# A spectral mixer's opening: near rows of the last DFT group summed and mirrored by DVE, the preceding tokens scaled by ACT

## The chip, the cores and the metric

The kernel runs on one core of one Trainium2 chip. The metric is the device time of one execution in microseconds (us); lower is better. The core's engines run side by side and are ordered by semaphores: TensorE (PE, with PEld for its weight loads), VectorE (DVE), ScalarE (ACT), GpSimd (POOL) and SyncE (SP), which issues the transfers here.

## What is computed

An input of 4 sequences of 3072 tokens with 256 channels goes through three stages: the real part of a DFT over tokens and channels, a channel mixing layer in which each token is blended with the one before it, and a routed layer of 8 experts.

```python
X = np.fft.fft(np.fft.fft(x, axis=1), axis=2).real              # 4 x 3072 x 256
x_prev = np.concatenate([zeros(B, 1, D), X[:, :-1, :]], axis=1)
xk = mu_k * X + (1.0 - mu_k) * x_prev
xr = mu_r * X + (1.0 - mu_r) * x_prev
v = np.maximum(xk @ w_k, 0.0) ** 2 @ w_v                         # 256 -> 1024 -> 256
x = sigmoid(xr @ w_r) * v
# then: per token the expert with the largest x @ w_gate, up to 384 tokens
# for each expert in order, out = prob * (relu(x @ w1[e]) @ w2[e])
```

## The kernel before

**Tiles and stages.** The 256 channels lie on 128 partitions in two halves, h = 0 and 1; tokens lie along the free dimension, in the tile `xt`. A sequence is 24 rows (`N2`) of 128 tokens, and a mixing tile is 512 tokens, so 4 rows (`NEAR`) of the sequence, 24 tiles in all. For the first sequence the whole DFT runs ahead of the first tile (`first_dft` of each engine); the DFTs of the other three are cut into pieces that run between the products of the tiles before them.

**Precision.** Matmul operands are float32 values split into a high part (rounded to the format of the fast matmul) and a low part (the rest). A product is three matmuls: high x high, weights' low x high, high x low. ACT makes the high part by copying `raw` to the narrower type (`high_part`, L745), DVE the low part by subtracting (`low_part`, L966).

**The last step of the DFT.** PE multiplies 13 blocks in four groups (`GROUPS3`, `step3`), each into an odd and an even bank. A block gives 5 (`JS`) token positions in each of the 24 rows. ACT copies the odd bank to `odd_copy`; DVE's `sums` (L946) adds it to the even bank for channel half 0 and subtracts for half 1. That gives positions 0 to 64 of each row. The other 63 are mirror images: `mirrors` (L699) on ACT copies half 1's positions in reverse to half 0 of the row at the other end and the reverse. `outer` picks the rows 0 to 3 and 20 to 23 (the near rows: rows 0 to 3 are the first tile, and rows 20 to 23 are their mirror images' sources), `inner` the 16 between. The channel that sits alone at the fold, partition 0 of half 1, comes from a separate small product, and SP writes it into `xt` by DMA (`place_edge`, L489): first its near rows once all near mirrors are done, later the others.

**The first tile.** With the near rows in place, DVE takes the difference between each token and its predecessor (L994, L956), multiplies it by mu and adds the predecessor (L1001, L963); ACT makes the high parts (L735, L737, L748), DVE the low ones (L969). Channel half 0 of xk is done in two halves of 256 tokens so that PE can start early. PE's `opening_ups` (L1404) computes the first four 128-wide blocks of the hidden layer in four banks, block by operand: high parts of xk half 0 (L1411), its low part (L1414), then the gate's products of xr half 0 (L1437), xk half 1 (L1422), and so on to L1430. Before the opening PE fills its wait with products of zeros (L385). After it come `up(4)` and `up(5)`, `down(0)`, `up(6)` and so on: each up writes a block of the hidden layer to a bank that its relu must have left (`hb_drained`), each down adds a block's contribution to the output. ACT's relu of the first block (L773) stands in its queue behind all mirrors of the first sequence. DVE squares what relu leaves (L1086) and makes its low part (L1081), ACT its high part (L768).

**What sets the order.** Each engine's program is written out by hand, and each engine runs it strictly in order; a wait holds everything behind it. Counting semaphores tie them together: `s3_summed` counts sums, `near_mirrored[h]` near mirrors of a half, `x_high` high parts, `mixed` low parts (one ahead), `hb_drained` relus (two ahead).

Of the kernel before, what the change touches and what calls it, by code (L numbers as in the profile page):

```python
# [18 lines left out]
P = 128  # L19
BATCH, SEQ, DIM, FF = 4, 3072, 256, 1024  # L20
EXPERTS, EFF = 8, 1024
N1, N2 = 128, 24
# [4 lines left out]
JS = 5  # L27
# [68 lines left out]
def build(nc, ins, out, cap):  # L96
# [55 lines left out]
    mu_r = ph("mu_r", [P, DH])  # L152
    earlier = ph("earlier", [P, P], bf16)
# [97 lines left out]
    half_dx, half_raw, half_high = sem("half_dx"), sem("half_raw"), sem("half_high")  # L251
# [38 lines left out]
    OPENING = [0, 2, 1, 3]  # L290
# [17 lines left out]
    first_quads, later_quads = [v_pair, h_pair, r_pair, v_pair], [r_pair, v_pair, r_pair, r_pair]  # L308
# [57 lines left out]
    def outer(rows):  # L366

        return rows.rearrange("p (b s) j -> p b s j", s=NEAR)[:, ::N2 // NEAR - 1]

# [107 lines left out]
    with ctx:  # L477
        with nc.Block("main") as block:
# [189 lines left out]
            def _(act):  # L668
# [42 lines left out]
                def first_dft():  # L711
# [191 lines left out]
            def _(dve):  # L903
# [67 lines left out]
                def first_dft():  # L971
# [14 lines left out]
                    for g in range(QUADS - 1):  # L986
                        sums(0, first_quads, g)
                    sums(0, first_quads, QUADS - 1, (1, 0))
                    dve.wait_ge(consts_in, 16 * CONSTS)
                    dve.wait_ge(s3_summed, DH * QUADS)  # L990
                    dve.wait_ge(near_mirrored[0], QUADS)
                    dve.wait_ge(mixed, 1)
                    for k, half in enumerate(HALVES):
                        dx = nc.vector.tensor_tensor(xr_raw[:, 0, half], xt[:, 0, half.start + 1:half.stop + 1], xt[:, 0, half], ALU.subtract)  # L994
                        if k == 0:
                            dx.then_inc(half_dx, 1)
                            dve.wait_ge(half_dx, 1)
                        else:
                            dx.then_inc(dx_ready, 1)
                            dve.wait_ge(dx_ready, 1)  # L1000
                        raw = nc.vector.scalar_tensor_tensor(xk_raw[:, 0, half], xr_raw[:, 0, half], mu_k[:, 0:1], xt[:, 0, half], ALU.mult, ALU.add)  # L1001
                        if k == 0:
                            raw.then_inc(half_raw, 1)
                        else:
                            raw.then_inc(raw_ready, 1)
                    dve.wait_ge(raw_ready, 1)
                    mix(0, OPENING[1], 0)
                    low_part(OPENING[0], 0, 0)
                    dve.wait_ge(near_mirrored[1], QUADS)
                    dve.wait_ge(near_edge_in, 32)  # L1010
                    difference(0, 1, 0)
                    mix(0, OPENING[2], 0)
                    low_part(OPENING[1], 0, 1)
                    low_part(OPENING[2], 0, 2)
                    mix(0, OPENING[3], 0)
                    low_part(OPENING[3], 0, 3)
# [244 lines left out]
            def _(pe):  # L1261
# [34 lines left out]
                def step3(seq, quads, g):  # L1296
# [5 lines left out]
                    for bank, lo, m, full3 in ((odd, 0, m_odd, s3_odd_full), (even, ZO, m_even, s3_even_full)):  # L1302
                        for q in range(*GROUPS3[g]):
                            at = (q - GROUPS3[g][0]) * SCOLS
                            done = mm(bank[:, at:at + SCOLS], z[:, q, lo:lo + P], m, start=True, stop=True)  # L1305
# [11 lines left out]
                def first_dft():  # L1317
# [9 lines left out]
                    for g in range(QUADS):  # L1327
# [6 lines left out]
                        step3(0, first_quads, g)  # L1334
# [6 lines left out]
                def route_rows(m):  # L1341
                    for h in range(DH):
# [313 lines left out]
```

## Time and profile before

| | |
|---|---|
| Median of 3 timed runs | 606.71 us (606.59 to 606.94) |
| The profiled execution | 607.38 us |
| Its span, first to last instruction | 605.5 us |
| PE busy | 595.1 us, 98% |
| DVE busy | 446.8 us, 74% |
| ACT busy | 319.2 us, 53% |
| POOL busy | 102.5 us, 17% |
| Chain that ended last | PE 91%, DMA 3%, DVE 2%, ACT 1% |

Times in rows are microseconds from the span's first instruction. A row of the timeline gives the start, the duration, the engine, the line, the operation, its output and inputs, the shapes, how many instructions are merged in it, and in brackets the engine's idle time before it with what ended it. SPq is a transfer being issued by SyncE. Instructions of one engine overlap a little: the next starts before the last one's end. A float32 product of the DFT is two PE records, as is a product of zeros. A mean over the whole span says little here, since the change touches 15 us of it.

### The profile page before, as it was taken

The numbers are of one execution on the slowest core, as the hardware profiler recorded it, in microseconds if no ns is written. First come the engines' busy times: TensorE is split into PE (matmuls) and PEld (weight loads), VectorE is DVE, ScalarE is ACT, GpSimd is POOL, SyncE is SP. The second block draws the span as 40 slices with busy tenths as digits, with TensorE's granted clock in tenths as the row PEclk, the third lists the DMA queues.
The fourth block names the chain that finished last, engine by engine and source line by source line (L and its number), as shares of the span: only waits on it lengthen the run. The fifth ranks groups of instructions, "written<-read, shape, count | busy, mean of one in ns | idle before, by whom it ended". The sixth has DMA issues, their size and how long they took to land.

```text
span 605.5 us, 9916 instructions
## 1 busy us (share of the span) xinstructions
PE 595.1 (98%) x3366; PEld 514.2 (85%) x3366; DVE 446.8 (74%) x1042; ACT 319.2 (53%) x725; POOL 102.5 (17%) x103
## 2 busy tenths in 40 slices
PE   8999999999999999999999999999999999999996
PEld 5978788888888888888888888888888999999996
DVE  4688888877777688888776767688885777766672
ACT  1674645554546563645444536564646555664450
POOL 0610302020202020202020202010205110111111
PEclk9999999999999999999999999999999999999999
DMA  8529936241510005202010100024104934455100
GB/s 302 159 75 217 394 133 206 91 142 53 185 52 23 2 11 198 93 0 64 3 37 1 34 1 5 29 70 169 31 1 156 348 115 138 164 194 175 44 28 27
DMA packets 42168, 63.14 MB, mean 104 GB/s; under 512 B 4582, under 2 KB 32055, under 8 KB 42108
## 3 DMA queue, kind: packets, MB, share of 16 engines
q1 hardware_dynamic: 38268, 55.88, 28.8%
q0 software_dynamic: 3840, 6.52, 3.0%
q8 instruction: 30, 0.49, 0.3%
q14 instruction: 30, 0.25, 0.1%
HBM read 39.90 MB, written 26.91 MB: 110 GB/s over the span
## 4 chain that ended last, share of the span: by engine, by line
PE 91%; DMA 3%; DVE 2%; issue 1%; SPq 1%; ACT 1%; POOL 0%; POOLq 0%; DVEq 0%; ACTq 0%
PE bank L303 69%; PE bank L1384 6%; PE bank L1349 4%; PE bank L1293 3%; PE bank L1305 2%; PE bank L1278 2%; DMA dispatched<-rows,slot 1%; DMA first_partner<-in_x 1%; PE bank L1576 1%; PE bank L1397 1%; DMA got<-dispatched 1%; DVE xt L952 0%; SPq L485 0%; PE bank L1593 0%; PE bank L1594 0%
## 5 line engine op out<-in xcount | busy, mean ns | idle before, releaser
L303 PE MATMUL bank<-k,wv 128*128 128x512 f32 x672 | 165.5, 396 | 0.0
L303 PEld LDWEIGHTS bank<-k,wv 128*128 128x128 f32 x672 | 125.5, 188 | 29.1
L303 PE MATMUL bank<-xk,wk 128*128 128x512 f32 x492 | 124.1, 398 | 0.0
L637 POOL DMA_INDIRECT dispatched<-rows,slot x56 | 61.0, 1089 | 361.3 <-DVE slot L1067 348.5
L303 PEld LDWEIGHTS bank<-xk,wk 128*128 128x128 f32 x492 | 91.2, 188 | 20.2
L773 ACT ACTIVATE relu<-bank 128x512 f32<-128x512 f32 x114 | 67.8, 597 | 74.6 <-PE bank L303 61.2
L1086 DVE TENSOR_TENSOR square<-relu 128x512 f32<-128x512 f32 x113 | 77.8, 691 | 39.0 <-ACT relu L773 25.3
L1081 DVE TENSOR_TENSOR k<-square,k 128x512 fp32r<-128x512 f32 x112 | 76.9, 686 | 2.8 <-ACT k L768 2.8
L768 ACT ACTIVATE k<-square 128x512 fp32r<-128x512 f32 x113 | 70.7, 626 | 11.7 <-DVE square L1086 11.4
L303 PE MATMUL bank<-down_w,he 128*128 128x256 f32 x576 | 72.0, 284 | 0.0
L303 PEld LDWEIGHTS bank<-down_w,he 128*128 128x128 f32 x576 | 70.4, 191 | 0.0
L1248 DVE SCALAR_TENSOR_TENSOR he<-bank,he 128x384 fp32r<-128x384 f32 x64 | 35.6, 557 | 37.7 <-ACT he L894 31.2
L894 ACT ACTIVATE he<-bank 128x384 fp32r<-128x384 f32 x64 | 31.4, 492 | 57.0 <-PE bank L303 29.9
L662 POOL DMA_INDIRECT out_rows<-ye,who x24 | 23.4, 974 | 111.7 <-DVE ye L1258 107.4
L1384 PE MATMUL bank<-xk,wk 128*128 128x512 f32 x144 | 41.3, 409 | 0.0
L303 PE MATMUL bank<-xr,wr 128*128 128x512 f32 x162 | 40.2, 396 | 0.0
L303 PEld LDWEIGHTS bank<-xr,wr 128*128 128x128 f32 x162 | 30.4, 188 | 7.0
L1100 DVE TENSOR_TENSOR x<-gate_r,bank 128x512 f32<-128x512 f32 x28 | 19.1, 687 | 18.7 <-PE bank L303 18.6
L754 ACT ACTIVATE rows<-bank 128x16 f32<-128x16 f32 x56 | 9.5, 184 | 42.6 <-PE bank L1349 41.5
L748 ACT ACTIVATE xr<-xr_raw 128x512 fp32r<-128x512 f32 x30 | 19.0, 632 | 24.4 <-DVE xr_raw L963 24.0
L303 PE MATMUL bank<-xe,up 128*128 128x384 f32 x168 | 29.8, 334 | 0.0
L303 PEld LDWEIGHTS bank<-xe,up 128*128 128x128 f32 x168 | 29.2, 188 | 0.0
(153 smaller groups left out, 800.0 us busy)
## 6 DMA issues: line engine op xcount, KB each, us to landing
out_rows<-blank SPq DMA_DIRECT2D x16, 768.0 KB, 4.4
raw_up<-in_moe_w SPq DMA_DIRECT2D x8, 1024.0 KB, 20.2
raw_down<-in_moe_w SPq DMA_DIRECT2D x8, 1024.0 KB
got<-dispatched SPq DMA_DIRECT2D x16, 409.5 KB, 3.0
x_area<-in_x SPq DMA_DIRECT2D x12, 384.0 KB
y<-in_x SPq DMA_DIRECT2D x9, 384.0 KB
dispatched<-blank SPq DMA_DIRECT2D x1, 3276.0 KB, 19.1
first_partner<-in_x SPq DMA_DIRECT2D x3, 384.0 KB
```

The costliest lines, as they stand in the source:

```text
L303: done = nc.tensor.matmul(bank, w, x, start=first and i == 0, stop=last and i == len(terms) - 1)
L637: nc.gpsimd.indirect_dma_start(out=slots_dram, out_offset=bass.IndirectOffsetOnAxis(ap=slot[:, g:g + 1], axis=0), in_=rows[:, g, :], in_of ...
L662: nc.gpsimd.indirect_dma_start(out=out, out_offset=bass.IndirectOffsetOnAxis(ap=who[:, i, j:j + 1], axis=0), in_=ye[:, i, j, :], in_offset ...
L768: nc.scalar.activation(k2_at(0, f), square[:, f % 2, :], ACT.Copy).then_inc(k2_high, 1)
L773: nc.scalar.activation(relu[:, f % 2, :], up_bank(n, f)[:, :], ACT.Relu).then_inc(hb_drained, 1)
L894: nc.scalar.activation(he[:, 0, f, :], hbe[f % 3][:, 0:cap], ACT.Relu).then_inc(he_high, 1)
L1081: nc.vector.tensor_tensor(k2_at(1, f), square[:, f % 2, :], k2_at(0, f).bitcast(fp32), ALU.subtract).then_inc(squared, 1)
L1086: nc.vector.tensor_tensor(square[:, f % 2, :], relu[:, f % 2, :], relu[:, f % 2, :], ALU.mult).then_inc(square_ready, 1)
L1100: nc.vector.tensor_tensor(x3[:, h, :], gate_r[:, h, :], vb[h][:, :], ALU.mult).then_inc(x3_done, 1)
L1248: nc.vector.scalar_tensor_tensor(he[:, 1, f, :], hbe[f % 3][:, 0:cap], 0.0, he[:, 0, f, :].bitcast(fp32), ALU.max, ALU.subtract).then_inc( ...
L1349: done = mm(tb[g][:, h * SPLIT:(h + 1) * SPLIT], x3[:, h, g * P:(g + 1) * P], fan[:, h, :], start=True, stop=True)
L1384: done = mm(hb[f % 2][:, :], *terms[k], start=k == 0, stop=k == len(terms) - 1)
```

## The change

Only the first sequence's last step and the first tile are touched.

The last group of `step3` writes its banks row by row (`in_rows`): the two blocks' 5 positions of a row stand side by side, so that a row is ten columns in one piece, and PE's output goes in steps of ten. Its even bank is now bank 7 (`lb`) and no longer the second of the pair `vb`. DVE makes, from the banks and `odd_copy`, the near rows and at once their mirror images (`near_sums`); the ACT mirrors of those rows are gone. The inner rows of the last group are summed at the end of the opening (`inner_sums`), and ACT mirrors them behind that.

The blend is computed another way: ACT multiplies the predecessor tokens by 1 - mu (`rest_k`, `rest_r`, made by two small DVE instructions) into `xk_raw` and `xr_raw`, counted by `part_ready`. DVE multiplies the tokens by mu and adds that product, once with the high part as its output (`mix_high`; three of the four high parts) and once again to give the raw value (`mix_part`), from which it subtracts the high part as before. The fourth high part (xr, half 1) is still made by ACT. The differences of the first tile are gone. PE multiplies two products of zeros, into bank 0, where it multiplied two and a half into bank 7.

```diff
-    first_quads, later_quads = [v_pair, h_pair, r_pair, v_pair], [r_pair, v_pair, r_pair, r_pair]
+    first_quads, later_quads = [v_pair, h_pair, r_pair, (vb[0], lb)], [r_pair, v_pair, r_pair, r_pair]
...
+    def by_rows(v, g):
+        width = (GROUPS3[g][1] - GROUPS3[g][0]) * JS
+        return v[:, 0:N2 * width].rearrange("p (s j) -> p s j", j=width)
...
                     copy_odd(0, first_quads, 3)
-                    mirrors(0, 2, outer, near_mirrored)
-                    mirrors(0, 3, outer, near_mirrored, (1, 0))
-                    act.wait_ge(half_raw, 1)
-                    nc.scalar.activation(xk[:, 0, 0, HALVES[0]], xk_raw[:, 0, HALVES[0]], ACT.Copy).then_inc(half_high, 1)
-                    act.wait_ge(raw_ready, 1)
-                    nc.scalar.activation(xk[:, 0, 0, HALVES[1]], xk_raw[:, 0, HALVES[1]], ACT.Copy).then_inc(x_high, 1)
-                    high_part(OPENING[1], 0, 1)
+                    mirrors(0, 2, outer, near_mirrored, (1, 0))
+                    act.wait_ge(rests, 2)
+                    act.wait_ge(near_mirrored[0], QUADS)
+                    for half in HALVES:
+                        nc.scalar.activation(xk_raw[:, 0, half], xt[:, 0, half], ACT.Copy, scale=rest_k[:, 0:1]).then_inc(part_ready, 1)
+                    nc.scalar.activation(xr_raw[:, 0, :], xt[:, 0, 0:TOK], ACT.Copy, scale=rest_r[:, 0:1]).then_inc(part_ready, 1)
+                    act.wait_ge(near_mirrored[1], QUADS)
+                    act.wait_ge(near_edge_in, 32)
+                    nc.scalar.activation(xk_raw[:, 1, :], xt[:, 1, 0:TOK], ACT.Copy, scale=rest_k[:, 1:2]).then_inc(part_ready, 1)
+                    nc.scalar.activation(xr_raw[:, 1, :], xt[:, 1, 0:TOK], ACT.Copy, scale=rest_r[:, 1:2]).then_inc(part_ready, 1)
                     mirrors(0, 1, inner)
-                    mirrors(0, 2, inner)
-                    high_part(OPENING[2], 0, 2)
-                    high_part(OPENING[3], 0, 3)
+                    high_part(3, 0, 3)
+                    mirrors(0, 2, inner, order=(1, 0))
                     mirrors(0, 3, inner, order=(1, 0))
...
+                def near_sums(quads, g):
+                    even = s3_banks(quads, g)[1]
+                    dve.wait_ge(s3_even_full, g + 1)
+                    dve.wait_ge(s3_odd_copied, g + 1)
+                    lo, hi = mirrored_js(g)
+                    for h in range(DH):
+                        op, other = ((ALU.add, ALU.subtract), (ALU.subtract, ALU.add))[h]
+                        halves = [outer(by_rows(v, g)) for v in (even, odd_copy[:, g % 2])]
+                        nc.vector.tensor_tensor(outer(rows_of(h, g)), *halves, op)
+                        nc.vector.tensor_tensor(outer(mirrored_rows_of(h, g)), *(v[..., 0:hi - lo] for v in halves), other).then_inc(near_mirrored[h], 1)
...
+                def inner_sums(quads, g):
+                    halves = [inner(by_rows(v, g)) for v in (s3_banks(quads, g)[1], odd_copy[:, g % 2])]
+                    for h in (1, 0):
+                        op = (ALU.add, ALU.subtract)[h]
+                        nc.vector.tensor_tensor(inner(rows_of(h, g)), *halves, op).then_inc(s3_summed, 1)
...
+                def mix_high(i, part):
+                    parts, raw, h = MIXED[i]
+                    dve.wait_ge(part_ready, part)
+                    nc.vector.scalar_tensor_tensor(parts[:, 0, h, :], xt[:, h, 1:TOK + 1], (mu_k if i < DH else mu_r)[:, h:h + 1],
+                                                   raw[:, h, :], ALU.mult, ALU.add).then_inc(x_high, 1)
...
+                def mix_part(i, high=0):
+                    _, raw, h = MIXED[i]
+                    if high:
+                        dve.wait_ge(x_high, high)
+                    else:
+                        dve.wait_ge(part_ready, len(MIXED) + 1)
+                    nc.vector.scalar_tensor_tensor(raw[:, h, :], xt[:, h, 1:TOK + 1], (mu_k if i < DH else mu_r)[:, h:h + 1],
+                                                   raw[:, h, :], ALU.mult, ALU.add).then_inc(raw_ready, 1)
...
-                    keep_warm(2)
-                    keep_warm_with(1, relu[:, 0, 0:P], relu[:, 1, HALVES[0]])
+                    pe.wait_ge(s3_summed, DH * 2)
+                    keep_warm_with(2, relu[:, 0, 0:P], relu[:, 1, :], hb[0])
                     pe.wait_ge(fan_in, 16 * 2 * DH)
                     pe.wait_ge(wk_split, len(WK_PIECES))
-                    pe.wait_ge(s3_summed, DH * QUADS)
+                    pe.wait_ge(s3_odd_copied, QUADS)
+                    pe.wait_ge(s3_summed, DH * (QUADS - 1))
```

The inner sums' completion is waited for by ACT's mirrors and, before the first routing product, by PE.

DVE's queue before, from the sums of the last group to the first low part; `xt` are the tokens, `xk_raw` and `xr_raw` the blends (and differences), and an output in `xk` or `xr` is a high or low part:

```order
L952 TENSOR_TENSOR xt<-bank,odd_copy 128x2x24x5 x2
L994 TENSOR_TENSOR xr_raw<-xt 128x256
L1001 SCALAR_TENSOR_TENSOR xk_raw<-xr_raw,mu_k,xt 128x256
L994 TENSOR_TENSOR xr_raw<-xt 128x256
L1001 SCALAR_TENSOR_TENSOR xk_raw<-xr_raw,mu_k,xt 128x256
L963 SCALAR_TENSOR_TENSOR xr_raw<-xr_raw,mu_r,xt 128x512
L969 TENSOR_TENSOR xk<-xk_raw,xk 128x512
```

The same stretch now:

```order
L973 TENSOR_TENSOR xt<-bank,odd_copy 128x2x4x10
L974 TENSOR_TENSOR xt<-bank,odd_copy 128x2x4x9
L973 TENSOR_TENSOR xt<-bank,odd_copy 128x2x4x10
L974 TENSOR_TENSOR xt<-bank,odd_copy 128x2x4x9
L1050 SCALAR_TENSOR_TENSOR xk<-xt,mu_k,xk_raw 128x256 x2
L1006 SCALAR_TENSOR_TENSOR xr<-xt,mu_r,xr_raw 128x512
L1016 SCALAR_TENSOR_TENSOR xk_raw<-xt,mu_k,xk_raw 128x512
L1022 TENSOR_TENSOR xk<-xk_raw,xk 128x512
```

Four short sums take the place of two long ones, the differences (L994) are gone, and between the first high parts (L1050) and the low part (L1022) stand a high part of xr (L1006) and a raw value (L1016).

DVE's queue before, from there to the first squares of the tile:

```order
L956 TENSOR_TENSOR xr_raw<-xt 128x512
L963 SCALAR_TENSOR_TENSOR xk_raw<-xr_raw,mu_k,xt 128x512
L969 TENSOR_TENSOR xr<-xr_raw,xr 128x512
L969 TENSOR_TENSOR xk<-xk_raw,xk 128x512
L963 SCALAR_TENSOR_TENSOR xr_raw<-xr_raw,mu_r,xt 128x512
L969 TENSOR_TENSOR xr<-xr_raw,xr 128x512
L1017 TENSOR_SCALAR next_slot<-small 128x8
L1018 TENSOR_SCALAR limit<-small 128x8
L1086 TENSOR_TENSOR square<-relu 128x512 x2
```

And now:

```order
L1006 SCALAR_TENSOR_TENSOR xk<-xt,mu_k,xk_raw 128x512
L1016 SCALAR_TENSOR_TENSOR xr_raw<-xt,mu_r,xr_raw 128x512
L1016 SCALAR_TENSOR_TENSOR xk_raw<-xt,mu_k,xk_raw 128x512
L1022 TENSOR_TENSOR xr<-xr_raw,xr 128x512
L1022 TENSOR_TENSOR xk<-xk_raw,xk 128x512
L1016 SCALAR_TENSOR_TENSOR xr_raw<-xt,mu_r,xr_raw 128x512
L1022 TENSOR_TENSOR xr<-xr_raw,xr 128x512
L980 TENSOR_TENSOR xt<-bank,odd_copy 128x16x10 x2
L1071 TENSOR_SCALAR next_slot<-small 128x8
L1072 TENSOR_SCALAR limit<-small 128x8
L1140 TENSOR_TENSOR square<-relu 128x512 x2
```

The difference (L956) is gone, one more high part (L1006) and one more raw value have come, and the inner sums (L980) stand behind the last low part, ahead of the squares.

ACT's queue before, from the last near mirrors to the first relu, with the semaphores it waits for:

```order
L703 ACTIVATE xt<-xt 128x2x4x9 [waits s3_summed] x2
L735 ACTIVATE xk<-xk_raw 128x256 [waits half_raw]
L737 ACTIVATE xk<-xk_raw 128x256 [waits raw_ready]
L748 ACTIVATE xr<-xr_raw 128x512 [waits raw_ready]
L703 ACTIVATE xt<-xt 128x16x20 [waits s3_summed] x2
L703 ACTIVATE xt<-xt 128x16x15 [waits s3_summed] x2
L748 ACTIVATE xk<-xk_raw 128x512 [waits raw_ready]
L748 ACTIVATE xr<-xr_raw 128x512 [waits raw_ready]
L703 ACTIVATE xt<-xt 128x16x9 [waits s3_summed] x2
L773 ACTIVATE relu<-bank 128x512 [waits square_ready,hb_full] x2
```

And now:

```order
L753 ACTIVATE xk_raw<-xt,rest_k 128x256 [waits near_mirrored_0,rests]
L753 ACTIVATE xk_raw<-xt,rest_k 128x256
L754 ACTIVATE xr_raw<-xt,rest_r 128x512
L757 ACTIVATE xk_raw<-xt,rest_k 128x512 [waits near_edge_in,near_mirrored_1]
L758 ACTIVATE xr_raw<-xt,rest_r 128x512
L720 ACTIVATE xt<-xt 128x16x20 [waits s3_summed] x2
L767 ACTIVATE xr<-xr_raw 128x512 [waits raw_ready]
L720 ACTIVATE xt<-xt 128x16x15 [waits s3_summed] x2
L720 ACTIVATE xt<-xt 128x16x9 [waits s3_summed] x2
L792 ACTIVATE relu<-bank 128x512 [waits square_ready,hb_full] x2
```

Five scalings (L753 to L758) stand where three copies to high parts stood; the one high part that is left (L767) comes ahead of the inner mirrors of the third and fourth group, and the relu behind them all as before.

## Rows read from the trace of the kernel before

**Rows 1.** The page: its head, and part 1, busy time of each engine.

```profile
span 605.5 us, 9916 instructions
...
PE 595.1 (98%) x3366; PEld 514.2 (85%) x3366; DVE 446.8 (74%) x1042; ACT 319.2 (53%) x725; POOL 102.5 (17%) x103
```

**Rows 2.** Chain that ended last, 29 to 58 us: start, us, what.

```profile
30.00 0.72 DVE xt L952 x2
...
31.52 0.49 DVE xk_raw L1001
...
32.04 0.42 ACT xk L735
...
32.60 2.14 PE bank L1411 x16
```

**Rows 3.** Waits of PE, 31 to 60 us: who waited for whom, us, times, longest.

```profile
PE bank L1411 <- ACT xk L735: 0.5, 1, 0.5
```

**Rows 4.** Timeline of DVE, the last DFT step and the first tile.

```profile
23.61 0.23 DVE L942 COPY x_area<-bank 120x65 f32<-120x65 f32 x1
23.75 0.22 DVE L943 TENSOR_TENSOR x_area<-bank,x_area 120x64 f32<-120x64 f32 x1
...
29.08 1.64 DVE L952 TENSOR_TENSOR xt<-bank,odd_copy 128x360 f32<-128x360 f32 x4 [0.86 <-PE bank L1305]
...
32.90 0.75 DVE L963 SCALAR_TENSOR_TENSOR xr_raw<-xr_raw,mu_r,xt 128x512 f32<-128x512 f32 x1
33.56 0.69 DVE L969 TENSOR_TENSOR xk<-xk_raw,xk 128x512 fp32r<-128x512 f32 x1
34.17 0.69 DVE L956 TENSOR_TENSOR xr_raw<-xt 128x512 f32<-128x512 f32 x1
```

**Rows 5.** Timeline of ACT, from the near mirrors to the later relus.

```profile
29.79 1.24 ACT L703 ACTIVATE xt<-xt 128x120 f32<-128x120 f32 x4
...
37.73 0.63 ACT L748 ACTIVATE xr<-xr_raw 128x512 fp32r<-128x512 f32 x1 [1.42 <-DVE xr_raw L963]
38.26 0.54 ACT L703 ACTIVATE xt<-xt 128x144 f32<-128x144 f32 x2
39.23 1.08 ACT L773 ACTIVATE relu<-bank 128x512 f32<-128x512 f32 x2 [0.42 <-PE bank L1427]
40.59 0.63 ACT L768 ACTIVATE k<-square 128x512 fp32r<-128x512 f32 x1 [0.27 <-DVE square L1086]
...
42.12 0.59 ACT L773 ACTIVATE relu<-bank 128x512 f32<-128x512 f32 x1
42.85 0.63 ACT L768 ACTIVATE k<-square 128x512 fp32r<-128x512 f32 x1
...
44.34 0.60 ACT L773 ACTIVATE relu<-bank 128x512 f32<-128x512 f32 x1
...
49.73 0.60 ACT L773 ACTIVATE relu<-bank 128x512 f32<-128x512 f32 x1 [1.68 <-PE bank L303]
```

**Rows 6.** Timeline of PE, the last DFT step and behind the first products.

```profile
26.89 0.62 PE L1314 MATMUL bank<-x_area,c_third_sb 120*24 120x13 f32 x10
27.44 2.49 PE L1305 MATMUL bank<-c_third_sb,x_area 120*128 120x120 f32 x20
...
34.58 1.08 PE L1414 MATMUL bank<-xk,wk 128*128 128x512 f32 x4
...
41.13 2.96 PE L303 MATMUL bank<-xk,wk 128*128 128x512 f32 x12
43.93 1.56 PE L303 MATMUL bank<-k,wv 128*128 128x512 f32 x6
45.33 1.56 PE L303 MATMUL bank<-xk,wk 128*128 128x512 f32 x6
```

**Rows 7.** Timeline of SyncE, the near edge rows.

```profile
31.11 0.76 SPq L490 DMA_DIRECT2D xt<-edge  x1
```

**Rows 8.** The DMA view, window 33.1 to 33.5 us.

```profile
DMA packets 8, 0.00 MB, mean 3 GB/s; under 512 B 8, under 2 KB 8, under 8 KB 8
```

More of the change, by code:

```diff
@@ L152, in build @@
     mu_r = ph("mu_r", [P, DH])
+    rest_k = ph("rest_k", [P, DH])
+    rest_r = ph("rest_r", [P, DH])
     earlier = ph("earlier", [P, P], bf16)
@@ L250, in build @@
     mixed = sem("mixed")
-    half_dx, half_raw, half_high = sem("half_dx"), sem("half_raw"), sem("half_high")
+    rests = sem("rests")
+    part_ready = sem("part_ready")
+    half_high = sem("half_high")
     wk_high = sem("wk_high")
@@ L289, in build @@
     MIXED = [(xk, xk_raw, 0), (xk, xk_raw, 1), (xr, xr_raw, 0), (xr, xr_raw, 1)]
-    OPENING = [0, 2, 1, 3]
     HALVES = [slice(0, TOK // 2), slice(TOK // 2, TOK)]
@@ L368, in outer, with rows_of, mirrored_rows_of @@
         return rows.rearrange("p (b s) j -> p b s j", s=NEAR)[:, ::N2 // NEAR - 1]
+    def by_rows(v, g):
+        width = (GROUPS3[g][1] - GROUPS3[g][0]) * JS
+        return v[:, 0:N2 * width].rearrange("p (s j) -> p s j", j=width)
+    def rows_of(h, g):
+        lo, hi = GROUPS3[g]
+        return by_s(h)[:, :, JS * lo:JS * hi]
+    def mirrored_rows_of(h, g):
+        return mirror(h, *mirrored_js(g))
     def inner(rows):
@@ L985, in first_dft @@
                     nc.vector.tensor_tensor(wr[:, 1, :, :], raw_wr[:, :, :], wr[:, 0, :, :].bitcast(fp32), ALU.subtract).then_inc(wr_split, 1)
-                    for g in range(QUADS - 1):
-                        sums(0, first_quads, g)
-                    sums(0, first_quads, QUADS - 1, (1, 0))
+                    sums(0, first_quads, 0)
+                    sums(0, first_quads, 1)
                     dve.wait_ge(consts_in, 16 * CONSTS)
-                    dve.wait_ge(s3_summed, DH * QUADS)
@@ L991, in first_dft @@
-                    dve.wait_ge(near_mirrored[0], QUADS)
+                    nc.vector.tensor_scalar(rest_k[:, :], mu_k[:, :], -1.0, 1.0, ALU.mult, ALU.add).then_inc(rests, 1)
+                    nc.vector.tensor_scalar(rest_r[:, :], mu_r[:, :], -1.0, 1.0, ALU.mult, ALU.add).then_inc(rests, 1)
+                    sums(0, first_quads, 2, (1, 0))
+                    near_sums(first_quads, 3)
+                    dve.sem_inc(dx_ready, DH)
                     dve.wait_ge(mixed, 1)
                     for k, half in enumerate(HALVES):
-                        dx = nc.vector.tensor_tensor(xr_raw[:, 0, half], xt[:, 0, half.start + 1:half.stop + 1], xt[:, 0, half], ALU.subtract)
+                        dve.wait_ge(part_ready, k + 1)
+                        high = nc.vector.scalar_tensor_tensor(xk[:, 0, 0, half], xt[:, 0, half.start + 1:half.stop + 1], mu_k[:, 0:1],
+                                                              xk_raw[:, 0, half], ALU.mult, ALU.add)
@@ L995, in first_dft @@
                         if k == 0:
-                            dx.then_inc(half_dx, 1)
-                            dve.wait_ge(half_dx, 1)
-                        else:
[L999 to L1005, printed above, removed]
@@ L1006, in first_dft @@
-                    dve.wait_ge(raw_ready, 1)
[L1007 to L1016, printed above, removed]
+                            high.then_inc(half_high, 1)
+                        else:
+                            high.then_inc(x_high, 1)
@@ new lines, in first_dft @@
+                    mix_high(2, 3)
+                    dve.wait_ge(half_high, 1)
+                    mix_part(0, 1)
+                    dve.wait_ge(raw_ready, 1)
+                    low_part(0, 0, 0)
+                    mix_high(1, 4)
+                    mix_part(2, 2)
+                    mix_part(1, 3)
+                    dve.wait_ge(raw_ready, 2)
+                    low_part(2, 0, 1)
+                    dve.wait_ge(raw_ready, 3)
+                    low_part(1, 0, 2)
+                    mix_part(3)
@@ L1017, in first_dft @@
+                    low_part(3, 0, 3)
+                    inner_sums(first_quads, 3)
                     nc.vector.tensor_scalar(next_slot[:, :], expert_no, float(cap), None, ALU.mult)
@@ L1294, in step2, with step3 @@
                         done.then_inc(full2, 1)
-                def step3(seq, quads, g):
+                def step3(seq, quads, g, in_rows=False):
+                    if in_rows:
+                        pe.wait_ge(s3_odd_copied, quads.index(v_pair) + 1)
                     pe.wait_ge(ze_ready, len(TRIPLES) * seq + [i for i, (lo, hi) in enumerate(TRIPLES) if lo < GROUPS3[g][1]][-1] + 1)
@@ L1304, in step3 @@
                             at = (q - GROUPS3[g][0]) * SCOLS
-                            done = mm(bank[:, at:at + SCOLS], z[:, q, lo:lo + P], m, start=True, stop=True)
+                            place = bank[:, at:at + SCOLS]
+                            if in_rows:
+                                place = bank.rearrange("p (s i j) -> p i s j", s=N2, j=JS)[:, q - GROUPS3[g][0]]
+                            done = mm(place, z[:, q, lo:lo + P], m, start=True, stop=True)
                         done.then_inc(full3, 1)
```

4 lines of the change are left out of this document (3 added, 1 removed).

## The prediction

> **What bounds the kernel now.** I read the page first: PE is busy for 98% of the 605.5 us span [rows 1], so an edit in the opening pays only by what it moves TensorE. The chain of waits says where that can be. Before 32.60 it runs through DVE's sums, differences and mixes and one ACT copy; from 32.60, the first matmul of L1411, it stays on PE [rows 2]. The list of PE's waits has one entry between 31 and 60 us, 0.5 us for that ACT copy [rows 3]. So the end moves with the moment at which PE gets through the opening, unless something that now has slack becomes late. The slack behind the opening is small: the fifth relu (L773) ends at 44.34 + 0.60 = 44.94, and the hidden products that reuse its bank start at 45.33 [rows 5, 6]. From a completed ACT instruction to the matmul it releases 0.14 us pass (32.04 + 0.42 = 32.46 to 32.60) [rows 2], so 0.25 us of slack remain there.
>
> **The front: near rows and the first high part.** The two tiny instructions for 1 - mu stand where DVE idles 0.86 us for PE [rows 4]; a copy of 65 columns takes 0.23 us there [rows 4], so they cost nothing. The sums of the last group took 0.72 us for 2 x 240 columns from 30.00 [rows 2]. Now DVE makes four instructions of 80 and 72 columns. From one start to the next are 0.14 us at 65 columns (23.61 to 23.75) [rows 4] and 0.36 at 240, so I take 0.16 each, and 0.24 until the last is done. The first half of the channels is ready at 30.00 + 0.16 + 0.24 = 30.40, the second at 30.72, and ACT's mirrors of that group (the last two of four, to 31.03) are gone [rows 5]. ACT scales 256 tokens from 30.44, 0.42 us by the copy of that size [rows 2], to 30.86; the hand-over to DVE takes 0.03; one scalar_tensor_tensor of 0.49 [rows 2] ends at 31.37; PE starts at 31.51 instead of 32.60: **1.09 us earlier**. Its warm-keeping products end about then.
>
> **What of it PE keeps.** L1411 needs 34.58 - 32.60 = 1.98 us [rows 2, 6] and is done at 33.49. Next PE needs the low part of half 0 of xk, which now stands behind two more steps. ACT's three scalings end at 31.71 (0.33 us apart at 256 columns, the third takes 0.63 as the copy of 512 does) [rows 5]. DVE makes the high part of xr from 31.74 and remakes raw xk from 32.41 (such steps start 0.66 apart, 32.90 to 33.56, and last 0.75); the low part runs from 33.20 and lasts 0.69 [rows 4]. PE gets it at 33.89 + 0.14 = 34.03, after a wait of 0.54. Against 34.58 this is **0.55 us earlier**. The 28 products up to L303 took 6.55 us without a wait (34.58 to 41.13) [rows 6], so PE arrives there at 40.58.
>
> **The edge rows.** SP issues them 0.08 us behind the last near mirror, at 31.11 [rows 7]; with that mirror at 30.72 it is 30.80. Packets still move in the window from 33.1 to 33.5 [rows 8], and L956, which needs the rows, starts at 34.17 without idle time [rows 4]: they land between about 33.2 and 34.17. I take 33.9, in the upper half, since the last packets move behind 33.1 and the completion has to follow them. After: 33.59 (bounds 32.9 and 33.9). ACT scales half 1 from 33.62 to 34.25, so that DVE, free at 33.81, makes the high part of xk half 1 from 34.28.
>
> **The tail of the opening, which sets the result.** From 34.28 DVE has three scalar_tensor_tensors (to 36.28), two low parts (0.61 apart, to 37.49) and the last mix, done at 38.24. ACT makes the last high part, 0.63, to 38.90. DVE subtracts from 38.93 and only then, at 39.54, makes the inner sums, two of 160 columns some 0.25 apart: ready at 39.86 and 40.10. On ACT their two mirrors stand ahead of the first relu, with 0.22 us between starts (two in 0.54) [rows 5]. The second starts at 40.13 and the first relu at 40.35, against 39.23 [rows 5]: **1.12 us later**. The parts that PE itself waits for are in time (x_high 3 at 35.0 against a need at 35.9; mixed 3 and 4 at 37.0 and 37.6 against 37.8 and 38.2). But up(4) needs the first relu, 40.35 + 0.60 + 0.14 = 41.09, where PE is at 40.58 (before: 41.13). Down(0) needs the fourth, 42.71 + 1.12 + 0.14 = 43.97 (before: 43.93). Up(6) needs the fifth, 44.94 + 1.12 + 0.14 = **46.20 against 45.33** [rows 5, 6]. Between the first and the fifth relu ACT pauses for 0.27 us for DVE's first square and for some 0.2 before 42.85 [rows 5]; both squares follow from a relu, so the shift comes through. Behind up(6) ACT waits for PE again (1.68 us at the relu of 49.73) [rows 5], and PE has no wait to 60 us [rows 3] that could take the 0.87 back. SP's second pair of edge rows, and the loads queued behind it, come later by the delay of the last mirrors; the pair's first reader is a difference behind the sixth relu of this tile, itself later.
>
> The sum: 606.71 + 0.87 = **607.6 us**. The profiled execution took 607.38 around its span of 605.5 [rows 1], 0.67 over the median; by its own kind the sum is 608.25. I stand on the median.
>
> **Bounds of what the trace does not show.** ACT with a scale from a tile: 0.60 to 0.63 us for 512 columns by the relus and copies [rows 5]; I take 0.63. In the Trainium skill, "ScalarE: Activation LUTs", section "What ACT_TABLE_LOAD costs", each such pointer operand adds about 93 ns to an ACTIVATE; no row here has one. By that page the scaling of half 1 ends 0.09 us later and the sum would be 607.7. Group 3 is now written to its banks in steps of ten columns. L1314 writes in steps of five, ten records in 0.62 us [rows 6], so I take 0; the far end is that each of the eight records (0.12 us each, 20 in 2.49 [rows 6]) takes twice as long, 0.9 us. Below nothing is excluded: no fewer columns are written. Edge rows: landing at 33.2 leaves DVE no wait, 0.47 us back (+0.40 in all); 34.17 gives +1.15. If ACT closes its pauses between the relus, up to 0.4 comes back.
>
> **The rivals.** (1) The gain is kept: PE's 0.55 reaches the end, 606.71 - 0.55 = 606.2. For it speaks that PE is the bound nearly everywhere; against it that the mirrors wait behind the inner sums. It needs the first relu by 38.9, so an edge at its early end, closed pauses and a quicker last mix together. Part of the way, early edge and closed pauses, gives 606.71 + 0.87 - 0.47 - 0.4 = 606.7. (2) The strided writes cost 0.9: near sums start later and all behind them, 0.87 + 0.9 = 1.77, 608.5. It decides from 0.34 us on, 0.04 a record; beyond that the kernel is slower by over 0.2%. (3) The work that DVE took over is itself the bound, whatever the waits: from 31.74 it has six scalar_tensor_tensors, four low parts, two inner sums and two small ones, 6 x 0.66 + 4 x 0.61 + 0.5 + 0.3 = 7.2 us, to 38.9. That is less than the 40.3 with its waits, so this alone gives no loss against now (39.3) and is the weakest.
>
> **How the numbers follow.** Forecast, with the edge rows anywhere in their bracket: 607.1 to 608.0, chance 0.68. Gain kept or part of it: 0.16. Strided writes or another late step: 0.14; DVE as such: 0.02. A measurement tells about 0.2%, 1.2 us, from no change. Faster than 605.5 has no mechanism here: 0.02. Slower than 607.9 is rival 2 and the top of the forecast: 0.21. Same: 0.77. The range, 606.2 to 608.2, leaves out most of rival 2 and little else.
>
> **What would show it.** Right: the first products of the opening start near 31.5; PE waits 0.5 us before the low products that follow; ACT idles some 2.7 us before the last high part and then waits for the inner sums at 39.9; the first relu starts at 40.3; PE waits for relus near 40.6 and 45.4. Wrong: a first relu before 39.5 (rival 1), near sums that start after 30.3 (rival 2), edge rows outside their bracket.

## The result and the profile after

The change makes the kernel slower by a third of a per cent, more than was predicted and in part for another reason.

| | before | after |
|---|---|---|
| Median of 8 timed runs | 606.68 us (606.43 to 607.08) | 608.66 us (607.98 to 609.08) |
| Ratio, 95% interval | | 1.0032 (1.0023 to 1.0041) |
| The profiled execution | 607.38 us | 608.54 us |
| Its span | 605.5 us | 606.7 us |

The profiled execution of before lay 0.7 us over its median, that of after at its own. So the two spans differ by only 1.2 us where the timed medians differ by 1.98.

The page of after, head and busy time of TensorE, against [rows 1]:

```profile
span 606.7 us, 9920 instructions
...
PE 595.2 (98%) x3364; PEld 512.9 (85%) x3364; DVE 448.3 (74%) x1048; ACT 319.5 (53%) x724; POOL 102.7 (17%) x103
```

**The opening.** Timeline of PE in after (start us, duration, engine, line, operation, count, and in brackets the idle time before with what ended it), against [rows 6] and the end of [rows 2]:

```profile
27.38 2.49 PE L1364 MATMUL bank<-c_third_sb,x_area 120*128 120x120 f32 x20
...
31.66 2.12 PE L1473 MATMUL bank<-xk,wk 128*128 128x256 f32 x16
34.16 1.20 PE L1476 MATMUL bank<-xk,wk 128*128 128x512 f32 x4 [0.38 <-DVE xk L1022]
...
40.80 3.04 PE L306 MATMUL bank<-xk,wk 128*128 128x512 f32 x12
43.86 1.64 PE L306 MATMUL bank<-k,wv 128*128 128x512 f32 x6
45.89 1.67 PE L306 MATMUL bank<-xk,wk 128*128 128x512 f32 x6 [0.39 <-ACT relu L792]
...
59.06 2.02 PE L1411 MATMUL bank<-fan,x 128*128 128x136 f32 x16
```

PE starts 0.94 us earlier than before (31.66 against 32.60), waits 0.38 us for the low part, is still 0.42 us ahead there (34.16 against 34.58), and comes to up(6) at 45.89 against 45.33: 0.56 us late, with a new wait for a relu. The list of PE's waits between 31 and 60 us had one entry [rows 3]; now it has these two:

```profile
PE bank L306 <- ACT relu L792: 0.4, 1, 0.4
PE bank L1476 <- DVE xk L1022: 0.4, 1, 0.4
```

The list shows less than half of what PE loses to the late relus. At up(4) it is 0.33 us ahead (40.80 against 41.13), at up(6) 0.56 late, so 0.89 us go in between. In the trace's single records neighbouring products start 0.23 us apart, but 0.32, 0.41, 0.31 and 0.78 us pass before those that start at 41.11, 43.86, 44.18 and 45.89, which is 0.9 us too much in all. Before has no such gap there.

Timeline of ACT in after, against [rows 5]:

```profile
30.41 0.91 ACT L753 ACTIVATE xk_raw<-xt,rest_k 128x256 f32<-128x256 f32 x2
31.22 0.71 ACT L754 ACTIVATE xr_raw<-xt,rest_r 128x512 f32<-128x512 f32 x1
33.32 0.72 ACT L757 ACTIVATE xk_raw<-xt,rest_k 128x512 f32<-128x512 f32 x1 [1.39 <-DMA xt<-edge]
...
38.06 0.63 ACT L767 ACTIVATE xr<-xr_raw 128x512 fp32r<-128x512 f32 x1 [2.65 <-DVE xr_raw L1016]
...
39.68 0.57 ACT L720 ACTIVATE xt<-xt 128x144 f32<-128x144 f32 x2 [0.38 <-DVE xt L980]
40.15 1.07 ACT L792 ACTIVATE relu<-bank 128x512 f32<-128x512 f32 x2
...
45.24 0.60 ACT L792 ACTIVATE relu<-bank 128x512 f32<-128x512 f32 x1
```

This is the tail as predicted: ACT idles 2.65 us for the last raw value, makes the last high part, waits again for the inner sums (L980), mirrors, and reaches the first relu at 40.15 instead of 39.23.

Timeline of DVE in after, against [rows 4]:

```profile
29.93 0.24 DVE L973 TENSOR_TENSOR xt<-bank,odd_copy 128x80 f32<-128x80 f32 x1
30.09 0.22 DVE L974 TENSOR_TENSOR xt<-bank,odd_copy 128x72 f32<-128x72 f32 x1
30.23 0.23 DVE L973 TENSOR_TENSOR xt<-bank,odd_copy 128x80 f32<-128x80 f32 x1
30.47 0.23 DVE L974 TENSOR_TENSOR xt<-bank,odd_copy 128x72 f32<-128x72 f32 x1
31.03 0.88 DVE L1050 SCALAR_TENSOR_TENSOR xk<-xt,mu_k,xk_raw 128x256 fp32r<-128x256 f32 x2 [0.32 <-ACT xk_raw L753]
...
38.72 0.69 DVE L1022 TENSOR_TENSOR xr<-xr_raw,xr 128x512 fp32r<-128x512 f32 x1 [0.70 <-ACT xr L767]
39.33 0.55 DVE L980 TENSOR_TENSOR xt<-bank,odd_copy 128x160 f32<-128x160 f32 x2
```

**Behind the opening.** That is not all of it. At the first routing product behind the first tile (L1349 before, L1411 after) the two traces are 0.66 us apart (58.40 and 59.06, the rows of before further down), and from there to 457 us PE waits as little as before (0.4 us in all against 0.5, both in the DFTs of the later sequences). Yet at the first small products of that change the distance is 1.68 us. Timeline of PE, first before, then after:

```profile
58.40 2.01 PE L1349 MATMUL bank<-fan,x 128*128 128x136 f32 x16
...
455.86 0.82 PE L1576 MATMUL bank<-small,got 128*128 128x128 f32 x6
...
471.36 0.88 PE L1576 MATMUL bank<-small,got 128*128 128x128 f32 x6 [0.38 <-DMA got<-dispatched]
```

```profile
457.54 0.82 PE L1638 MATMUL bank<-small,got 128*128 128x128 f32 x6
...
472.58 0.82 PE L1638 MATMUL bank<-small,got 128*128 128x128 f32 x6
```

A further 1.0 us comes between 59 and 457 us, a little at a time, in code that the change doesn't touch. About 0.5 us of the whole is given back at 471 us, where before waits 0.38 us for a DMA and after doesn't; from there the distance stays at 1.2 us. The steady part can be seen in any tile. The 36 products of six downs in a row, and the row behind them, before and then after:

```profile
103.99 8.53 PE L303 MATMUL bank<-k,wv 128*128 128x512 f32 x36
112.35 0.63 PE L1384 MATMUL bank<-xk,wk 128*128 128x512 f32 x2
```

```profile
104.81 8.56 PE L306 MATMUL bank<-k,wv 128*128 128x512 f32 x36
113.21 0.62 PE L1446 MATMUL bank<-xk,wk 128*128 128x512 f32 x2
```

From the first of the 36 to the next row are 8.36 us before and 8.40 after, 232.2 and 233.3 ns a product, with no wait and at the same granted clock. I call this the pace. As a mean over all neighbouring 128x512 products of one kind between 60 and 440 us, worked out from the trace's records (pairs up to 245 ns apart), it is 232.6 ns before and 233.3 after. Some 1360 such records lie in that stretch, so 0.7 ns each is 0.9 us.

### The profile page after: what moved, and what is told of

The parts are those of the page before. It is cut to its first block, busy times and chain, and to the rows that moved or that the text cites. A ratio compares the mean times of both kernels' runs of the same rounds, so it can differ in the third digit from the quotient of the medians.

```text
span 606.7 us, 9920 instructions
## 1 busy us (share of the span) xinstructions
PE 595.2 (98%) x3364; PEld 512.9 (85%) x3364; DVE 448.3 (74%) x1048; ACT 319.5 (53%) x724; POOL 102.7 (17%) x103
## 4 chain that ended last, share of the span: by engine, by line
PE 92%; DVE 2%; issue 2%; ACT 2%; SPq 1%; DMA 1%; POOLq 0%; ACTq 0%; DVEq 0%
PE bank L306 71%; PE bank L1446 6%; PE bank L1411 4%; PE bank L1347 3%; PE bank L1364 2%; PE bank L1332 2%; DMA first_partner<-in_x 1%; PE bank L1638 1%; PE bank L1459 1%; PE bank L1655 0%; PE bank L1656 0%; PE bank L1659 0%; DVE square L1140 0%; SPq L502 0%; SPq L513 0%
## 5 line engine op out<-in xcount | busy, mean ns | idle before, releaser
L767 ACT ACTIVATE xr<-xr_raw 128x512 fp32r<-128x512 f32 x29 | 18.3, 633 | 25.6 <-DVE xr_raw L999 22.5
```

## The experiments

**Theory A**: the two new tiles `rest_k` and `rest_r`, 32 bytes a partition each, stand behind `mu_r` and move every tile behind them 64 bytes up in SBUF, `xt`, `xk`, `xr` and `k` among them, while the weights stay; this costs about 1 us in the pace, and the tail of the opening costs the other. **Theory B**: it is the place of the code (other instructions on PE ahead of the loops), or the order of the first tile that disturbs something later. **Theory C**: the drift belongs to the two profiled executions and not to the kernels. Every kernel here computes the whole result. Each ratio is against before on the same chip, with the 95% interval.

**Before with the two tiles, unused**

```diff
     mu_r = ph("mu_r", [P, DH])
+    rest_k = ph("rest_k", [P, DH])
+    rest_r = ph("rest_r", [P, DH])
```

> The kernel before with two small tiles declared behind mu_r that nothing uses, so that every tile from there to the end of the first phase lies 64 bytes higher, as in the changed kernel. Theory A (the place of the operands sets the pace of the 512-column products): they start 233.4 ns apart on average instead of 232.5, and the kernel takes about 1.2 us more, 607.9. Theory B (the place of PE's instructions does): no difference, 606.7. Theory C (the drift came from the profiled executions, not from the kernels): no difference, 606.7.

607.74 us against 606.63, 1.0017 (1.0008 to 1.0026): 1.1 us slower, with not one instruction changed. Pace 233.2 ns, that of after.

**After with the two tiles declared last**, behind every tile that TensorE reads

```diff
-    rest_k = ph("rest_k", [P, DH])
-    rest_r = ph("rest_r", [P, DH])
...
     first_need = ph("first_need", [P, NTILE + 1], i32)
+    rest_k = ph("rest_k", [P, DH])
+    rest_r = ph("rest_r", [P, DH])
```

> The changed kernel with its two small tiles declared last, so that all others lie where they lay before. Theory A: pace back to 232.5 ns, 608.66 - 1.2 = 607.4; what is left over the kernel before, 0.7, is the late relu chain. Theory B and C: 608.7.

607.42 us, 1.0013 (1.0004 to 1.0022). Pace 232.7, that of before; timeline of PE:

```profile
26.93 2.49 PE L1364 MATMUL bank<-c_third_sb,x_area 120*128 120x120 f32 x20
...
58.59 2.02 PE L1411 MATMUL bank<-fan,x 128*128 128x136 f32 x16
...
104.19 8.52 PE L306 MATMUL bank<-k,wv 128*128 128x512 f32 x36
112.55 0.62 PE L1446 MATMUL bank<-xk,wk 128*128 128x512 f32 x2
```

Without the shift the change costs 0.8 us; with the 1.1 of the run above that makes 1.9, and 1.98 were measured. The order of the first tile is that of after, and the pace is still that of before, so the second half of theory B falls; theory C falls with the timed medians of this run and the one above.

The 0.8 us can be seen in the opening, though not from the first routing product alone (58.59 against 58.40), since the profiled executions reach the last DFT group at different moments (26.93 here, 27.44 before, 27.38 in after). From the start of that group to the first routing product pass 30.96 us before, 31.66 here and 31.68 in after: the opening costs 0.7 us in both kernels with the late relus.

**After with two more instructions on PE**, which do no work

```diff
+    spare = sem("spare")
...
+                pe.sem_inc(spare, 1)
+                pe.sem_inc(spare, 1)
                 pe.wait_ge(warmer, 1)
```

> The changed kernel with two empty PE instructions (semaphore increments) ahead of its first product, so that PE's later code lies where it lay before (it is two instructions shorter in the changed kernel). Theory B: pace back to 232.5 ns, 607.4. Theory A and C: 608.7.

608.73 us, 1.0034 (1.0021 to 1.0048): as after. With it falls the first half of theory B, the place of the code.

**The tail**: the kernel with the tiles last, inner sums ahead of the last low part, and the third group's inner mirrors ahead of the last high part

```diff
+                    mirrors(0, 2, inner, order=(1, 0))
                     high_part(3, 0, 3)
-                    mirrors(0, 2, inner, order=(1, 0))
...
                     mix_part(3)
+                    inner_sums(first_quads, 3)
                     low_part(3, 0, 3)
-                    inner_sums(first_quads, 3)
```

> As the kernel with the two tiles last, and in the opening DVE makes the inner sums in its 0.7 us wait for the last high part, ahead of the last low part, and ACT mirrors the third group's inner rows ahead of that high part, where it idles for 2.65 us. My theory of the opening (the first relu is late since its queue waits for inner sums and four mirrors): first relu at 39.1 instead of 40.15, no wait of PE before up(6), and 1.0 to 1.1 us less than the kernel with the two tiles last. Rival (the relu chain is late for another reason, or PE would wait anyway for what DVE took over): less than 0.3 us off.

606.43 us, 0.9998 (0.9989 to 1.0007), 1.0 us less than with the tiles last alone. ACT's and PE's timelines in it:

```profile
38.09 0.63 ACT L767 ACTIVATE xr<-xr_raw 128x512 fp32r<-128x512 f32 x1 [2.02 <-DVE xr_raw L1016]
38.63 0.54 ACT L720 ACTIVATE xt<-xt 128x144 f32<-128x144 f32 x2
39.06 1.06 ACT L792 ACTIVATE relu<-bank 128x512 f32<-128x512 f32 x2
```

```profile
27.42 2.49 PE L1364 MATMUL bank<-c_third_sb,x_area 120*128 120x120 f32 x20
...
44.99 1.56 PE L306 MATMUL bank<-xk,wk 128*128 128x512 f32 x6
...
58.06 2.01 PE L1411 MATMUL bank<-fan,x 128*128 128x136 f32 x16
```

The last mirrors no longer wait for DVE, the relu comes at 39.06, and PE's waits between 31 and 60 us keep only the one for the low part. Up(6) starts at 44.99: 0.90 earlier than in after, 0.34 earlier than before. From the last DFT group to the first routing product pass 30.64 us, 1.0 less than with the tiles last alone and 0.3 less than before; that last bit is too little for the timed runs to tell from nothing. So the wait that took back the opening's gain is the one that the prediction named.

**How far the address matters.** In before, the weights `wk`, `wv` and `wr` start at 96 modulo 256 bytes (63584, 79968, 96352) and what they are multiplied with, `xk`, `xr` and `k`, at 224 (155872, 164064, 180448). Their distance is 128 modulo 256, and also modulo 512; in after it is 192. (The addresses follow from the order and the sizes of the tiles.) The next kernels are before with an unused tile in one place.

```diff
     mu_r = ph("mu_r", [P, DH])
+    ph("apart_128", [P, 32])
```

> The kernel before with every tile behind mu_r 128 bytes higher (no other change). Theory A1 (the pace of the 512-column products depends on where the moving operands lie against the weights, modulo 128 bytes): as before, 232.5 ns and 606.7. Theory A2 (any move away from the old places costs, by something longer than 128 bytes): 233.3 ns or more, 607.8.

599.79 us against 606.66, 0.9892 (0.9877 to 0.9907): 6.9 us faster, which neither expectation had. Timeline of PE:

```profile
102.42 8.32 PE L304 MATMUL bank<-k,wv 128*128 128x512 f32 x36
110.58 0.62 PE L1385 MATMUL bank<-xk,wk 128*128 128x512 f32 x2
```

8.16 us or 226.7 ns a product; the mean pace is 227.6. 5.0 ns on 1360 products are 6.8 us.

Weights and all behind them moved together, by 64 bytes:

```diff
+    ph("ahead_of_wk", [P, 16])
     wk = ph("wk", [P, 2, DH, FF], fp32r)
```

> The kernel before with 64 bytes ahead of wk: weights and moving operands both move by 64 bytes and keep their distance. If the distance between weights and moving operands matters: 232.5 ns, 606.7. If the moving operand's own place modulo 128 matters: 233.3 ns, 607.8.

606.56 us, 1.0001 (0.9992 to 1.001), pace 232.4: as before, though `xk`, `xr` and `k` stand where they stand in after. So the place of these tiles alone doesn't set the pace; the distance to the weights fits.

The same with 32 bytes behind `mu_r` (`ph("apart_32", [P, 8])`):

> The kernel before with every tile behind mu_r 32 bytes higher, so that the moving operands start at a multiple of 64 bytes (they start 32 bytes behind one in both kernels). If a start at a multiple of 64 or 128 is what the engine likes: pace under 232.5 ns, time under 606.7. If only the distance of 64 does harm: between the two, 606.7 to 607.8.

608.38 us, 1.0033 (1.0021 to 1.0045), pace 234.1 ns, the slowest pace found; the time lies above what either reading allowed.

**Another order in the first tile**, on top of the tail: the low part of xk half 0 ahead of the high part of xr, the last raw value earlier.

```diff
-                    high_part(3, 0, 3)
+                    high_part(3, 0, 2)
...
-                    mix_high(2, 3)
                     dve.wait_ge(half_high, 1)
                     mix_part(0, 1)
                     dve.wait_ge(raw_ready, 1)
                     low_part(0, 0, 0)
+                    mix_high(2, 3)
                     mix_high(1, 4)
                     mix_part(2, 2)
-                    mix_part(1, 3)
+                    mix_part(3)
                     dve.wait_ge(raw_ready, 2)
                     low_part(2, 0, 1)
-                    dve.wait_ge(raw_ready, 3)
+                    mix_part(1, 3)
+                    dve.wait_ge(raw_ready, 4)
                     low_part(1, 0, 2)
-                    mix_part(3)
```

> As the kernel with the tail reordered (e4), and DVE makes the low part of xk half 0 before the high part of xr, and the last raw value ahead of the raw value of xk half 1. By my theory of the opening PE loses its 0.4 us wait for that low part, the last high part and with it the first relu come 0.3 us earlier (38.8), and the kernel takes 0.3 us less than e4, 606.1. Rival (PE waits for mixed 3 or 4 instead, which come 0.1 to 0.2 later): the same as e4, 606.4.

606.43 us, 0.9995 (0.9986 to 1.0004). A miss: the same time as with the tail alone. Timeline of PE:

```profile
33.62 1.10 PE L1476 MATMUL bank<-xk,wk 128*128 128x512 f32 x4
...
38.18 1.21 PE L1489 MATMUL bank<-xk,wk 128*128 128x512 f32 x4 [0.20 <-DVE xk L1022]
...
44.80 1.55 PE L306 MATMUL bank<-xk,wk 128*128 128x512 f32 x6
```

PE no longer waits for the first low part (33.62 against 34.20 with the tail alone), but now for the low part of xk half 1; at up(6) 0.19 us are left (44.80 against 44.99), too little for the timed runs to show.

**After at distance 0** (modulo 256): 64 bytes more behind the two tiles (`ph("apart_64", [P, 16])`).

> The changed kernel with 64 bytes more behind its two small tiles, so that all later tiles lie 128 bytes above the kernel before, as in e5 (its moving operands then start at a whole multiple of 256 bytes from the weights). If the pace depends on that distance alone: 227.2 ns, and the time is e5's 599.8 plus what the opening costs, 0.7: 600.5. If the changed kernel were slow for another reason: over 602.

600.86 us against 606.58, 0.9904 (0.9888 to 0.9921), pace 227.7.

**The tail at distance 0** (`ph("apart_128", [P, 32])` behind `mu_r`):

> e4 (the changed kernel with the opening's tail reordered) with all tiles behind mu_r 128 bytes higher. Both effects add: e4 less 6.9, 599.5, 0.3 under e5 and about 1.0 under the changed kernel at the same place. If the faster products leave less slack for the first relu's chain, it loses some of that: 599.8.

599.54 us, 0.9884 (0.9868 to 0.9901), 1.3 us below after at the same distance. With the next one it is the fastest found.

**Distance 0 elsewhere**: before with the weights 64 and the others 192 bytes up (`ahead_of_wk` and `apart_128` together).

> The kernel before with 64 bytes ahead of wk and 128 behind mu_r: weights 64 and moving operands 192 bytes higher, so that their distance is again a whole multiple of 256, as in e5, at other places. If the distance modulo 256 decides: 227.2 ns, 599.8. If the place of the moving operands themselves decides (they stood 96 bytes behind a multiple of 256 in e5, now 160): about 232 to 234 ns, 606.5 to 608.5.

599.49 us, 0.9886 (0.9869 to 0.9902), pace 227.6, with weights and operands at other addresses than in the +128 kernel and the same distance.

**192 bytes**, distance 64 (`ph("apart_192", [P, 48])`):

> The kernel before with every tile behind mu_r 192 bytes higher: distance to the weights 64 modulo 256 (known: 0 gives 227.2 ns, 128 232.5, 160 234.0, 192 233.3). If the pace is set by how far two positions are apart in a circle of 256, this mirrors 192: 233.3 ns, 607.7. If only a distance of 0 is quick, but others differ in no order: anything from 230 to 235.

602.20 us, 0.9926 (0.991 to 0.9943), pace 229.3: quicker than either reading allowed.

**One operand alone**: 128 bytes ahead of `relu`, so that `k` stands at distance 0 and `xk` and `xr` stay at 128.

```diff
+    ph("ahead_of_relu", [P, 32])
     relu = ph("relu", [P, 2, TOK])
```

> The kernel before with 128 bytes ahead of relu, so that k2, the moving operand of the down products, lies at a whole multiple of 256 from its weights wv, while xk and xr stay where they are, 128 off theirs. If each product's own pair of operands sets its pace: down products 227.4 ns, hidden and gate products 232.5, and about half of e5's gain, 603.2. If something common to all products does (the place of the tiles that DVE and ACT read and write, say): both kinds alike, at 227 or at 232.5.

603.69 us against 606.66, 0.9948 (0.9931 to 0.9964): 3.0 of the 6.9 us that all three pairs gave, with 588 of the 1360 products. Timeline of PE, six products of an up, then 36 of downs:

```profile
102.58 1.55 PE L304 MATMUL bank<-xk,wk 128*128 128x512 f32 x6
103.97 8.34 PE L304 MATMUL bank<-k,wv 128*128 128x512 f32 x36
112.14 0.62 PE L1385 MATMUL bank<-xk,wk 128*128 128x512 f32 x2
```

The up's six take 1.39 us, 231.7 ns each, the downs 8.17 for 36, 226.9 ns. In the means: `k` with `wv` 228.5, `xk` with `wk` 232.3, `xr` with `wr` 232.0. So it is mainly a product's own pair that sets its pace. `k` with `wv` takes 232.7 ns before and 227.5 with all three pairs at distance 0, so moving `k` alone brings 4.2 of 5.2 ns; where the last 1.0 comes from stays open.

**160 bytes**, distance 32 (`ph("apart_160", [P, 40])`):

> The kernel before with every tile behind mu_r 160 bytes higher: distance to the weights 32 modulo 256. Known now: 0 gives 227.6 ns, 64 229.3, 128 232.6, 160 234.1, 192 233.3. If the pace falls off with the distance on from 0: about 228.5 ns, 601. If 0 and 64 are quick because both start 32 bytes behind a multiple of 64, as the weights do, and 160 is slow because it does not: slower than at 64, over 602.2.

607.55 us, 1.0014 (1.0005 to 1.0024), pace 233.4: slow, though it is nearer to 0 than the kernel at 64. So the pace doesn't fall off steadily with the distance.

| Distance modulo 256 (modulo 512) | pace, ns | kernels |
|---|---|---|
| 0 (256) | 227.6 to 227.7 | before +128; after +64; tail +128; before, both moved |
| 32 (288) | 233.4 | before +160 |
| 64 (320) | 229.3 | before +192 |
| 128 (128) | 232.4 to 232.7 | before; tiles last; tail; other order; both +64 |
| 160 (160) | 234.1 | before +32 |
| 192 (192) | 233.2 to 233.3 | after; before with the tiles; two more on PE |

Kernels at one distance agree within 0.3 ns, so the 0.7 ns between before and after is more than their scatter. The period isn't shown: no two kernels share a distance modulo 256 and differ modulo 512. Every distance called 0 here is 256 modulo 512, and what a multiple of 512 would give was not run.

Left open, besides the period: why 64 is quick and 192 and 32 are slow, what in the chip makes the difference, and whether operands other than these split 128x512 products care. The experts' tiles were not moved against their weights.

## Why the prediction was wrong

**The front was right, with one term too small.** Predicted for PE's first products 31.51, measured 31.66. The four near sums started 0.14 to 0.24 apart against 0.16, and ACT began at 30.41 against 30.44. ACT's scalings were under-sized: 0.71 and 0.72 us at 512 columns where a copy of that size takes 0.63 (L767), and 0.51 where 0.42 was taken at 256. I put the difference down to the scale read from a tile; no run here takes it away. The Trainium skill, "ScalarE: Activation LUTs", section "What ACT_TABLE_LOAD costs", gives about 93 ns for each such operand. The trace agrees, with 0.08 to 0.09 us. DVE made the first high part from 31.03, 0.14 later than worked out.

**The wait for the low part** was 0.38 us against 0.54, at 34.16 against 34.03: right.

**Strided writes** cost nothing: the 20 records of the last two groups, eight of which now write in runs of five columns that start ten apart, take 2.49 us as before, and the near sums start at 29.93. Rival 2 falls, and although the time is close to the 608.5 that it gave, its mechanism isn't there.

**The edge rows** were issued at 30.79 (30.80 predicted), and ACT, which waited for them, started at 33.32 instead of 33.62, inside the bracket. The taken value, from the upper half of the bracket of before, was 0.3 too late. DVE had no wait for ACT there; its last mix ended at 38.02 instead of 38.24.

**The tail** was right in kind and order: high part, low part, inner sums, mirrors, relu. The first relu came at 40.15 (40.35 predicted) and ACT's pauses did not close: from the first to the fifth relu it took 5.09 us, against 5.11 before. Up(6) came 0.56 us late and not 0.87, the rest of the difference being the edge rows' 0.2 and a hand-over from relu to PE shorter than taken (0.05 us from the end of the fifth relu, 45.24 + 0.60, to 45.89, against 0.14). With the tiles out of the way the opening cost 0.8 us at the end, and mending the tail's order gave 1.0 back.

**The step that failed** is "So the end moves with the moment at which PE gets through the opening", and, behind up(6), that PE has no wait to 60 us that could take the 0.87 back. It looked for waits behind the opening and took the products there as unchanged. Two tiles of 32 bytes, which the changed kernel declares in two lines and to which the prediction gave no price, slowed the 128x512 products by 0.7 ns each on average: 1.1 us at the end of the kernel. The opening's 0.8 and the tiles' 1.1 make up the 1.98 within 0.1. The first alone would have been 607.5, in the predicted range; the sum is 0.5 us above it. No rival of the prediction was a cost outside the opening.

**The base** was taken rightly: before's eight runs have a median of 606.68 against the 606.71 shown, so nothing of the miss comes from there.

## What to carry to other kernels

A diff that declares a tile moves every tile behind it, and a TensorE-bound kernel can pay for that in each product: put new small tiles last, or pad so that moving operand and weights keep their distance in bytes (the period isn't known, so a distance that is only equal modulo 256 may not do), and compare the time from one product to the next in a stretch that the change doesn't touch. Where TensorE is at 98% busy with one shape, try a few distances between the operands; one padding tile brought 1.1% here, more than the whole opening could. The change itself, with its tail mended, isn't shown to be worth anything: 606.43 us against 606.63, and at distance 0 599.54 against the 599.79 and 599.49 of the kernel before. When steps are moved in front of an in-order queue, look for what then stands between the last input and the first consumer: two instructions exchanged on each of two engines were worth 1.0 us.

## What the runs showed of the hardware

The time from one 128x512 product to the next depended on the distance in SBUF between the moving operand and the weights. Written modulo 512 bytes it was 227.6 ns at 256, 229.3 at 320, 232.6 at 128, 233.3 at 192, 233.4 at 288 and 234.1 at 160; whether the pattern repeats after 256 bytes was not measured. It was the same at one distance (0 modulo 256) for two placements of the weights (96 and 160 modulo 256). The granted clock was 0.997 or more in every timed run. The busy time of a single product in the rows is longer than the pace, since neighbouring products overlap, but moves with it: k with wv has a mean of 396 ns in before, 397 in after and 391 in before with the 128 bytes behind `mu_r`. A difference of 0.7 ns is easily missed there and adds up in the starts.

An ACT instruction with its scale in a tile took 0.71 to 0.72 us at 512 columns against 0.63 for a copy. TensorE wrote PSUM in runs of five columns that start ten apart as quickly as in one piece (20 records in 2.49 us in both kernels). A small SBUF transfer issued at 30.79 and 31.59 (two pieces) released its reader at 33.32.
